# Transform, gated feed-forward and cosine feed-forward on one core: five rows for means, an earlier second weight load, a later store and later mixings

## What is computed

```python
X = np.fft.fft(np.fft.fft(x, axis=1), axis=2).real     # x: 2 x 3008 x 256
x = X.reshape(6016, 256)
xn = x / np.sqrt(mean(x * x, -1) + 1e-6) * rms_g
x = (silu(xn @ w_gate) * (xn @ w_val)) @ w_out          # 256 -> 1536 -> 256
h = x @ w_in                                           # 256 -> 2048
out = (h * np.cos(h)) @ w_out2                         # 2048 -> 256
```

## Time and profile before

| | us |
|---|---|
| median of 3 runs | 994.25 |
| lowest, highest | 991.92, 999.22 |
| the profiled execution | 996.86 |
| its span | 995.0 |
| TensorE busy in it | 978.2 (98%), 4518 matmuls |
| VectorE, ScalarE, GpSimd busy | 743.5, 639.0, 351.2 |

### The profile page before, as it was taken

How to read it: one execution, slowest core, us unless ns; L and a number is a source line. 1 busy time by engine, 2 the same in 40 slices (tenths; PEclk the granted TensorE clock), 3 DMA queues, 4 the chain that set the end, 5 groups by cost and what they waited for, 6 DMA issues and landing times.

```text
span 995.0 us, 13011 instructions
## 1 busy us (share of the span) xinstructions
PE 978.2 (98%) x4518; PEld 813.3 (82%) x4518; DVE 743.5 (75%) x1028; ACT 639.0 (64%) x803; POOL 351.2 (35%) x292
## 2 busy tenths in 40 slices
PE   8988899999999999999999999999999999999998
PEld 8976688888888888888888888888888888888886
DVE  6868779668877668887767887667887767887665
ACT  5577568775448775348775438776347776437777
POOL 0368568007650006751005661004771003761000
PEclk9989999999999999999999999999999999999999
DMA  9776401001010001010001010000000000100001
GB/s 323 183 189 148 169 0 42 11 1 42 1 32 11 1 0 42 0 31 10 0 0 41 0 31 10 0 0 27 16 7 25 0 0 0 42 0 0 0 0 41
DMA packets 14082, 36.80 MB, mean 37 GB/s; under 512 B 2618, under 2 KB 6682, under 8 KB 13658
## 3 DMA queue, kind: packets, MB, share of 16 engines
q1 hardware_dynamic: 11978, 31.63, 9.4%
q0 software_dynamic: 2064, 4.72, 2.6%
HBM read 22.35 MB, written 9.26 MB: 32 GB/s over the span
## 4 chain that ended last, share of the span: by engine, by line
PE 91%; DMA 4%; DVE 2%; SPq 1%; POOL 1%; issue 0%; ACT 0%; DVEq 0%; ACTq 0%; POOLq 0%
PE ps L540 30%; PE ps L542 29%; PE ps L541 29%; DMA win_raw<-win 2%; PE ps L491 1%; DMA x_sb<-x 1%; DMA stat<-mean_row 1%; PE ps L509 1%; PE ps L507 1%; POOL work L1186 0%; SPq L320 0%; DVE plus L994 0%; DVE w_f L955 0%; DVE x_sb L885 0%; PE ps L477 0%
## 5 line engine op out<-in xcount | busy, mean ns | idle before, releaser
L540 PE MATMUL ps<-h_hi,wo_hi 128*128 128x502 f32 x672 | 262.9, 391 | 4.5 <-DVE h_lo L979 4.5
L542 PE MATMUL ps<-h_hi,wo_lo 128*128 128x502 f32 x672 | 262.4, 390 | 0.0
L541 PE MATMUL ps<-h_lo,wo_hi 128*128 128x502 f32 x672 | 262.2, 390 | 0.0
L1097 POOL TENSOR_TENSOR h_lo<-work,h_hi 128x502 fp32r<-128x502 f32 x92 | 101.8, 1114 | 377.3 <-ACT h_hi L781 369.9
L766 ACT ACTIVATE h_hi<-work 128x502 fp32r<-128x502 f32 x132 | 82.5, 626 | 176.9 <-POOL work L1186 176.7
L1084 DVE SCALAR_TENSOR_TENSOR work<-work,ps 128x1004 f32<-128x1004 f32 (+1 forms) x109 | 117.2, 1075 | 95.5 <-ACT work L863 95.1
L540 PEld LDWEIGHTS ps<-h_hi,wo_hi 128*128 128x128 f32 x672 | 126.9, 189 | 31.8 <-DVE h_lo L979 4.5
L1070 DVE SCALAR_TENSOR_TENSOR work<-work,ps 128x1004 f32<-128x1004 f32 (+1 forms) x109 | 116.5, 1074 | 48.0 <-ACT work L849 48.0
L540 PE MATMUL ps<-x_hi,win_hi 128*128 128x502 f32 x384 | 149.9, 390 | 0.0
L541 PE MATMUL ps<-x_lo,win_hi 128*128 128x502 f32 x384 | 149.4, 389 | 0.0
L542 PE MATMUL ps<-x_hi,win_lo 128*128 128x502 f32 x384 | 149.4, 389 | 0.0
(11 more groups left out here) (89 smaller groups left out, 1283.4 us busy)
## 6 DMA issues: line engine op xcount, KB each, us to landing
out<-y_sb SPq DMA_DIRECT2D x10, 502.0 KB, 3.3
x_sb<-x SPq DMA_DIRECT2D x6, 768.0 KB, 10.4
w_lo<-w_f POOLq DMA_DIRECT2D x6, 512.0 KB, 7.1
uv_t<-uv_dram SPq DMA_DIRECT2D x6, 502.0 KB, 3.5
wo_raw<-wo SPq DMA_DIRECT2D x1, 2048.0 KB, 9.6
win_raw<-win SPq DMA_DIRECT2D x1, 2048.0 KB, 19.6
raw_b<-w1b SPq DMA_DIRECT2D x3, 512.0 KB, 13.3
raw_a<-w1a SPq DMA_DIRECT2D x3, 512.0 KB, 14.0
```

Of the source, the lines that this page charges most:

```text
L540: nc.tensor.matmul(acc, w_hi, v_hi, start=start, stop=False)
L541: nc.tensor.matmul(acc, w_hi, v_lo, start=False, stop=False)
L542: return nc.tensor.matmul(acc, w_lo, v_hi, start=False, stop=stop)
L1097: nc.gpsimd.tensor_tensor(dst, src, hi.bitcast(F32), ALU.subtract).then_inc(s, 1)
```

## The change

- `mean_row` gets five rows, so a copy waits for the spread of the mean five before it. The seventh copy moves from `uv_copy` 15 to 14.
- The two late mixings move from the first tile into steps 31 and 32 of the transform.
- `wo1` is loaded on SP right behind the second mean's spread, ahead of the first inverse roots. The split of its first chunk moves from `uv_copy` 15 to 11, that of the fourth chunk of `w1` from 11 to 15; GpSimd's issues follow (`wo1_add(0)` before `add_squares(7)`, `w1_add(3)` behind it).
- SP waits for the second accumulating transfer (`w1_lo_done[1]`) before it stores the rest of the first batch.
- The spread of the last mean moves behind the load of `win2`, and with that `wo2` and the second batch's store no longer stand behind it. Its copy on ScalarE moves ahead of the first late split of `wo1`.

```diff
--- before.py
+++ after.py
@@ -120,7 +120,7 @@
         assert 4 * XCOLS <= o_o2l - o_i2h
         MEAN_COLS = max(max(p) for p in PARTS) * N2
         assert MEAN_COLS <= 512
-        SQUARES, ROWS = 4, 2
+        SQUARES, ROWS = 4, 5
         squares = sb("squares", [SQUARES, 2, MEAN_COLS], o_o2h)
         ROUNDS = (max(max(p) for p in PARTS) + 3) // 4
         mean_row = sb("mean_row", [ROWS, ROUNDS * N2], o_i2h + WO1B)
@@ -232,7 +232,7 @@
             return b * STEPS + k.stop - 1
 
         RMS_AT = [8, 9, 15, 20, 24, 28, 32]
-        MEAN_COPY_AT = [2, 3, 7, 9, 11, 13, 15]
+        MEAN_COPY_AT = [2, 3, 7, 9, 11, 13, 14]
         RMS_LATE = range(len(RMS_AT), MEANS)
         LAST_MEAN_AT = 3
         assert len(RMS_LATE) == 2
@@ -266,12 +266,11 @@
 
         W1_ORDER = [0, 3, 1, 4, 2, 5]
         SCALE_AT = [2, 6, 10, 19, 23, 28]
-        MIX_AT = [3, 5, 8, 9, 16, 18, 20, 22, 24, 26]
-        MIX_LATE = [10, 11]
-        W1_SPLIT_AT = {3: 0, 4: 1, 9: 2, 11: 3}
+        MIX_AT = [3, 5, 8, 9, 16, 18, 20, 22, 24, 26, 31, 32]
+        W1_SPLIT_AT = {3: 0, 4: 1, 9: 2, 15: 3}
         W1_NEGATE_AT = {12: 0, 15: 1}
         W1_EARLY = len(W1_NEGATE_AT)
-        WO1_SPLIT_AT = {15: 0}
+        WO1_SPLIT_AT = {11: 0}
         W1_SPLIT_LATE, WO1_SPLIT_LATE = {1: 4, 2: 5}, {3: 1, 4: 2}
         LATE_WIN2 = [7, 8]
         WIN2_ORDER = [0, 4, 1, 5, 2, 6, 3, 7]
@@ -383,6 +382,8 @@
             spread_mean(0)
             store_uv(0, (slice(0, 1), slice(1, FIRST_ROWS)))
             spread_mean(1)
+            sp.wait_ge(n1_done, 2 * NG)
+            load(wo1_raw[:, :], wo1, wo1_in)
             sp.wait_ge(uv_stored, UV_FIRST)
             sp.wait_ge(pq_done, STEPS)
             sp.wait_ge(inv_done, 1)
@@ -392,13 +393,12 @@
             load_inv(0)
             load_u128(0)
             spread_mean(2)
-            sp.wait_ge(n1_done, 2 * NG)
-            load(wo1_raw[:, :], wo1, wo1_in)
             spread_mean(3)
+            sp.wait_ge(w1_lo_done[1], 16)
             store_uv(0, (slice(FIRST_ROWS, K1 - 1), slice(K1 - 1, K1)))
             spread_mean(4)
             sp.wait_ge(uv_stored, UV_BATCH)
-            for q in STAT_MEANS[2]:
+            for q in STAT_MEANS[2][:-1]:
                 spread_mean(q)
             sp.wait_ge(uv_done, LAST)
             load(wo2_raw[:, :], wo2, wo2_in)
@@ -406,6 +406,7 @@
             for n in range(W1_CHUNKS):
                 sp.wait_ge(w1_lo_done[n], 16)
             load(win2_raw[:, :], win2, win2_in)
+            spread_mean(MEANS - 1)
             sp.wait_ge(inv_done, 2)
             store_inv(0, (slice(FIRST_ROWS, K1 - 1), slice(K1 - 1, K1)), sum(TAKE[:FIRST_ROWS]))
             sp.wait_ge(inv_out, INV_OUT[1])
@@ -807,12 +808,12 @@
                     if first and i == 0:
                         square(MEANS - 1)
                         mean_copy(RMS_LATE[0])
+                    if first and i == LAST_MEAN_AT:
+                        mean_copy(RMS_LATE[1])
                     if first and i in W1_SPLIT_LATE:
                         split_w1(W1_SPLIT_LATE[i])
                     if first and i in WO1_SPLIT_LATE:
                         split_wo1(WO1_SPLIT_LATE[i])
-                    if first and i == LAST_MEAN_AT:
-                        mean_copy(RMS_LATE[1])
                     if first and 6 <= i < 10:
                         if i == 6:
                             act.wait_ge(win2_in, 16)
@@ -1033,9 +1034,6 @@
                         dve.wait_ge(uv_stored, UV_BATCH)
                     if 0 < i < C1 - 1:
                         lo1(t, i - 1, 0)
-                    if first and i == 1:
-                        for k in MIX_LATE:
-                            mix_w1(k)
 
                 i = C1 - 1
                 for g in range(2):
@@ -1160,9 +1158,9 @@
             scale_u128(0)
             w1_add(2)
             add_squares(6)
+            wo1_add(0)
+            add_squares(7)
             w1_add(3)
-            add_squares(7)
-            wo1_add(0)
 
             def wo2_part(k):
                 c = slice(k * 512, (k + 1) * 512)
```

## The result

| | us |
|---|---|
| before, median (lowest to highest) | 994.56 (991.92 to 999.22) |
| after, median of 4 runs (lowest to highest) | 984.30 (984.04 to 984.61) |
| ratio, 95% interval | 0.9892 (0.9855 to 0.9929) |
| span of the profiled execution, before and after | 995.0 and 982.5 |
| TensorE busy in it | 978.2 and 972.3 |

The change takes 10.3 us off the median and 12.5 us off the profiled span. The spread is narrower too: 7.3 us between the four runs of before, 0.6 us between those of after.

The account below looks back on a forecast made before the run. TensorE, never idle from 125 us on, was taken as the bound, with time to win between 55 and 120 us. Gains of 3.7, 2.2, 1.3 and 5.9 sum to 13.1 us: 995.6 - 13.1 = 982.5 us, range 978 to 990.

Parts of the forecast that it names:

- A: TensorE's 1.75 us stop at 56.4 us and half clock behind it: shorter stop, clock stays up, gain 3.7 us.
- the restart at 57.6: TensorE resumes the means at 57.6 us, released by GpSimd's sum of squares, after 1.2 us idle instead of 1.75.
- Rival 2: Clock falls again behind the stop near 57 us in the changed kernel: 3.1 us lost, 985.6 us, chance 0.22.
- The clock: Behind the stop near 57 us, an idle time of 1.2 us was taken to keep the clock at full.
- B: Steps 1 to 3 of the first tile: three TensorE waits for VectorE go with the moved mixings, gain 2.2 us.
- C: TensorE's 1.17 us idle at 88.38 for the last mean's copy, behind a split of wo1: gain 1.3 us.
- D: TensorE's 4.04 us idle at 115.82, under ScalarE's wait for win2, and half clock after it: gain 5.9 us.
- the claim that with win2 in before 96.5 nothing is lost: win2, forecast in at 94, was to be early enough for ScalarE's rounding if landed by 96.5: no loss.
- the root's wait: ScalarE stands some 3 to 4 us before the root, for the last mean's spread queued behind win2; costed at nothing.
- Store of the first batch: Issued about 53.5, taken as 10 us, landing at 63.5 (62.5 to 68.6): cost 0, at most 1.9 us.
- Second accumulating transfer: Its landing, which the first moved mixing waits for: 53.5 us, between 51.7 and 59.95, hurting from 57.0; cost 0.
- The signs: Profile marks: no TensorE idle over 1.5 us, full clock 58 to 66, win2 issued near 84, landed by 96.5.

Follow-up runs that it names:

- undo_rows: The changed kernel with two rows for means instead of five: 984.66 us.
- rows_only: The kernel before with only five rows for means instead of two: 994.16 us, ratio to before 0.999.
- after_again: The changed kernel itself, run and profiled again: 984.54 us, with before beside it at 993.72.
- undo_copy: The changed kernel with the last mean's copy back behind the late split of wo1: 983.97 us.
- undo_spread: The changed kernel with the last mean's spread back ahead of the load of wo2: 989.99 us.
- best: The changed kernel with last mean's spread ahead of win2, seventh square and GpSimd's sum of squares earlier, last two mixings a step later: 985.07 us.
- no_store_wait: The changed kernel without SP's wait for the second accumulating transfer of w1 before the first batch's store: 984.45 us.

## Why the prediction was right, and where not

- **The range and the direction.** Forecast 982.5 us, 978 to 990; measured 984.3. The gain was 10.3, not 13.1, off by 2.8. That the forecast is off by only 1.8 is luck in part: it started from 995.6, 1.0 us above the measured median of before. Taken from the profiled execution alone, which all the rows came from, 996.9 - 13.1 = 983.8 was closer.
- **A, 3.7 us.** The restart at 57.6 was right (57.55), and so was its new cause, the sum of squares; the other half began at 61.42, forecast 61.5. The sixth copy came in time, but because of the early load: undo_rows has it in time with two rows. What failed is the step from the profiled execution to the median. I took the middle between 996.9 and 994.25 and kept the whole term, though the half clock of the earlier trace rows was the very thing that made that execution slower. In the second profile of before A is worth 0.00. So A is worth 3.7 in one execution of before and nothing in another, and the median of before (994.56) lies nearer the second (993.47) than the first (996.86). Rival 2 was a chance of the changed kernel in my text; it was one of the kernel before.
- **The clock.** "1.2 us lies between the idle time that kept the clock (1.17) and the one that lost it (1.75)" was the wrong kind of argument: 1.26 us lost it in rows_only and kept it in the changed kernel, 1.47 kept it in after_again. The Trainium skill (TensorE: Matmul & The Clock Gate, section "HAM oscillation — how this bites in real kernels") ties the loss of the clock to idle gaps and tells of gaps that a transfer makes again and again; here two kernels with the same single stop of 1.26 us came out on both sides, so for this stage the rule doesn't decide, and the measurement does. What decided there stays open.
- **B, 2.2 us.** 2.5 in the table; the three idle times were gone and came back when the mixings did. The moved mixings took 1.16 and 1.42 us at steps 31 and 32, inside the 0.74 to 1.75 that I gave, and held up nobody.
- **C, 1.3 us.** 1.46 in the table, but half of the reason was wrong: 0.75 of it came with the shift of the other engines, and the 0.71 of the copy's new place are not in the end result, since undo_copy isn't longer.
- **D, 5.9 us.** The cause was right, shown by undo_spread. The table gives 12.15 - 7.63 = 4.5 net. The changed kernel's own new waits take back the rest: the row of best, which has no idle time of TensorE behind 80 us, falls by 0.32 + 1.03 = 1.35 between 144 and 240, that of undo_copy by 0.71 + 0.64, the same, and 4.5 + 1.35 = 5.9. The mis-sized step is the claim that with win2 in before 96.5 nothing is lost. The last accumulating transfer took 7.4 us, win2 was issued at 85.73 and landed at 95.1, below that limit. But ScalarE's root went only at 96.12, when the spread queued behind win2 was in, and TensorE, expected at 99, came for the rounding at 98.58 and stood 0.20 us; the wait in the tenth item had no term at all. I had named the root's wait and costed it at nothing.
- **The transfers.** Store of the first batch: I took 10 us after an issue at 53.5; its large piece took 3.9 after 53.73, its last 4.1. Second accumulating transfer: landing at 53.5, measured 53.7. wo1, issued at 36.42, took 6.8 us, was in long before the rest of the first batch's store went out, and the first accumulating transfer beside it took 6.8 us against 6.1 before.
- **The signs.** Of those that I had named for being right, all came but one: a wait of TensorE on VectorE of more than 0.3 us after step 2, the 0.39 at 109.81. Win2 was issued 1.7 us later than named.
- **Parts that do nothing.** Five rows, the wait ahead of the store, and the copy's place could each be undone without loss; undoing them together wasn't tried. I had given the first of them the whole of A, and the last the whole of C.

## What to carry to other kernels

A long load queued behind other bulk pays for all of it: find what SP is waiting for in front of the bulk (here a 1.9 KB spread), move that wait behind it, and then ask what now lands behind the last load. A profile that shows a stretch of half clock behind a short stop is one draw among several; profile the kernel before twice, and count such a stretch in the forecast of the median only by how often it occurs. And when a change has six parts, undo them one by one: here two were undone with a loss, of 3.4 and 5.45 us, and three without. The changed kernel gained 9.2 us beside those two runs, so little is left for the sixth, the early load of wo1 with its shifted splits, in a median; it was tried alone, but not undone.

## What the runs showed of the hardware

- Behind stops of TensorE of 1.06 to 1.47 us among the small matmuls at the end of the transform, the granted clock stayed at 1.00 in ten profiles (in best with the stop two operations later) and fell to 0.50 in one (rows_only); behind 1.75 and 2.87 us it fell in both. Why it fell in some executions of one kernel and in none of 13 of another with the same stop stays open.
- A VectorE subtraction of two SBUF operands that takes 1.21 us took 3.26 in best, where GpSimd had begun a transfer's issue 0.27 us before it and a scaling followed. The Trainium skill (SBUF — State Buffer, section "SBUF: two separate sides") has a VectorE operation with two inputs in SBUF and a GpSimd one that reads SBUF shut each other out, whichever starts first. The length here would fit two GpSimd instructions going ahead of the VectorE one, although the second was recorded as begun 0.5 us later than it; no run separates the two.
- A store of 940 KB took 3.9 us in the changed kernel, where the next accumulating transfer was issued only 1.7 us behind it, 7.7 where one of 0.5 MB was already under way (no_store_wait), and 11.7 in the kernel before, beside such a transfer and behind 1.5 MB of load.
- A load of 2 MB took 9.4 us in the changed kernel and 20.1 in undo_spread, where 2 MB of load and 1.4 MB of store were issued up to 3.7 us ahead of it.
